# A retention layer with two mixers on one core: evictions of the up projection moved ahead of splits, two weight slots exchanged, one weight load moved ahead of the returning sum, first loads gated

## What is computed

```python
# retention, per head h
state = gamma[h] * state + outer(k[t], v[t]);  y[t] = scale * q[t] @ state
# mixer
theta = x @ w_theta
u = x + einsum('ts,bsd->btd', w_tok_r, x * cos(theta)) + einsum('ts,bsd->btd', w_tok_i, x * sin(theta))
x = u + maximum(u @ w_ch, 0)
# MLP
h = maximum(x.transpose(0, 2, 1) @ w_tok1, 0) @ w_tok2
u = x + h.transpose(0, 2, 1)
out = u + maximum(u @ w_ch1, 0) @ w_ch2          # d_ch = 1536
```

## Time and profile before

| | us |
|---|---|
| median of 3 runs | 440.97 (439.33 to 441.27) |
| the profiled execution | 443.38 |
| span of its trace, first to last instruction | 441.4 |
| TensorE busy in that span | 423.1 |
| VectorE busy | 309.3 |
| ScalarE busy | 179.0 |
| GpSimd busy | 115.6 |

### The profile page before, as it was taken

One profiled execution on the slowest core, in us unless ns is written; L12 is line 12 of the kernel. 1 busy time (PEld: TensorE's weight loads), 2 busy tenths in 40 slices (PEclk: granted clock), 3 DMA queues, 4 the chain that ended last, 5 costly groups with the idle time before them and its releaser, 6 DMA issues.

```text
span 441.4 us, 7037 instructions
## 1 busy us (share of the span) xinstructions
PE 423.1 (96%) x2820; PEld 399.6 (91%) x2820; DVE 309.3 (70%) x428; ACT 179.0 (41%) x273; POOL 115.6 (26%) x107
## 2 busy tenths in 40 slices
PE   6899999999999999999999979988999969999997
PEld 4687887899999999999989969989999959999997
DVE  2699997889999995244417872658456459999951
ACT  1336653654354546111312356133336163555500
POOL 1422240100210005996520035297341000000000
PEclk9999999999999999999999998999999999999999
DMA  8946779520495012001010600010023945530111
GB/s 300 405 153 252 299 174 234 108 72 25 120 209 196 6 46 96 2 31 65 0 49 15 246 26 0 1 48 1 0 73 113 314 108 97 126 103 9 63 71 73
DMA packets 12480, 47.78 MB, mean 108 GB/s; under 512 B 1185, under 2 KB 3361, under 8 KB 10657
## 3 DMA queue, kind: packets, MB, share of 16 engines
q1 hardware_dynamic: 9488, 33.03, 20.1%
q0 software_dynamic: 2816, 14.16, 14.4%
q10 hardware_dynamic: 144, 0.14, 0.1%
HBM read 41.04 MB, written 6.29 MB: 107 GB/s over the span
## 4 chain that ended last, share of the span: by engine, by line
PE 87%; DVE 5%; DMA 4%; ACT 2%; issue 2%; DVEq 0%; ACTq 0%
PE ps L1236 76%; PE ps L1253 3%; PE ps L1293 3%; DMA w_raw<-ch 3%; PE ps L1307 2%; PE ps L1384 1%; PE ps L1267 1%; DVE h_ops_c L1138 1%; DMA qkv_in<-qkv 1%; PE ps L1283 1%; DVE prob L882 1%; DVE u_sum L1065 1%; ACT u_a L751 0%; ACT u_b L751 0%; DVE w_sq L866 0%
## 5 line engine op out<-in xcount | busy, mean ns | idle before, releaser
L1236 PE MATMUL ps<-tw,zs 128*128 128x384 f32 x504 | 88.1, 335 | 0.0
L1236 PEld LDWEIGHTS ps<-tw,zs 128*128 128x128 f32 x504 | 87.4, 188 | 0.1
L1236 PE MATMUL ps<-h_ops_c,w_even 128*128 128x384 f32 x288 | 50.6, 334 | 0.0
L1236 PEld LDWEIGHTS ps<-h_ops_c,w_even 128*128 128x128 f32 x288 | 50.0, 188 | 0.0
L1236 PE MATMUL ps<-u_a,w 128*128 128x384 f32 x210 | 41.2, 340 | 4.0 <-DVE h_a L1107 3.1
L1236 PEld LDWEIGHTS ps<-u_a,w 128*128 128x128 f32 x210 | 37.2, 191 | 4.5 <-issue 4.5
L1236 PE MATMUL ps<-u_b,w 128*128 128x384 f32 x210 | 40.7, 339 | 0.0
L689 ACT ACTIVATE zs<-z 128x768 fp32r<-128x768 f32 x28 | 23.7, 846 | 36.9 <-PE ps L1236 36.9
L1236 PEld LDWEIGHTS ps<-u_b,w 128*128 128x128 f32 x210 | 37.6, 192 | 0.0
L1236 PE MATMUL ps<-ut,w_sq 128*128 128x384 f32 x192 | 35.5, 338 | 0.0
L1236 PEld LDWEIGHTS ps<-ut,w_sq 128*128 128x128 f32 x192 | 33.0, 188 | 0.0
(11 more groups left out here) (142 smaller groups left out, 781.7 us busy)
## 6 DMA issues: line engine op xcount, KB each, us to landing
qkv_in<-qkv SPq DMA_DIRECT2D x11, 1024.0 KB, 6.5
raw<-tok POOLq DMA_DIRECT2D x7, 1152.0 KB, 9.2
stage<-weights SPq DMA_DIRECT2D x11, 512.0 KB, 3.3
w_raw<-ch POOLq DMA_DIRECT2D x6, 768.0 KB, 6.8
cols_out<-res SPq DMA_DIRECT2D x2, 1536.0 KB, 5.2
total<-cols_out SPq DMA_DIRECT2D x4, 768.0 KB, 10.5
cols_out<-total SPq DMA_DIRECT2D x16, 192.0 KB, 1.8
raw<-tok SPq DMA_DIRECT2D x6, 384.0 KB, 7.1
```

The costliest lines, as they stand in the source:

```text
L1236: mm = pe.matmul(dst, left(l), right(r), start=first and n == 0, stop=last and n == 2, skip_group_check=True)
```

## The change

Line numbers behind the first hunk shift by a few; names are used from here on.

- **Evictions ahead of splits.** On VectorE, `sum_u(0, 3)` comes before `u_low(0, 4)`; in the first pair `sum_u(1, 2)` moves behind both `add_p7`; in every pair `second_units(m, 0, 1)` moves behind `add_p7` and `second_units(m, 1, 1)` behind `add_p2`. On ScalarE, `u_high(0, 5)` moves ahead of `keep_p1`, `u_high(1, 0)` ahead of `keep_p5`, and `u_high(1, 4)`, `(1, 5)`, `(1, 6)` behind both `first_units(m, 1, 1)`.
- **Operands of the down projection.** `h_op(0, 0)` is made at the start of pair 2 and `h_op(0, 1)` at the start of pair 3, each with its `h_sums(5, phi)`; before, both stood in the middle of pair 2 on ScalarE and at its start on VectorE. `h_sums(5, 2)` and `(5, 3)` move from the last pair into the first down product. `h_op_high(0, 0)` and `(0, 1)` get a wait on `u_lo[1]`, GpSimd's five splits.
- **Slots.** The slices of `w1` change places, and so do `w2_even` and `w2_odd`. With that `w2_raw1` lies over a part of the last slice's weights that only its products j = 1 and 2 read.
- **Second down weights.** SP loads `w2_raw1` after j = 2 of the last pair, ahead of the four blocks of `total`.
- **First loads.** SP waits for q and k of chunk 0 before it issues `theta_w`, for k and v of chunk 0 before chunk 2, and for chunk 1 before the third of `tok`.

```diff
--- before.py
+++ after.py
@@ -183,9 +183,9 @@
             u_b1 = sb("u_b1", [P, 4, 2, S], F32R, within=middle)
 
 
+        w2_odd = sb("w2_odd", [P, 2, W2C], F32R)
+        w2_raw1 = sb("w2_raw1", [P, W2C])
         w2_even = sb("w2_even", [P, 2, W2C], F32R)
-        w2_raw1 = sb("w2_raw1", [P, W2C])
-        w2_odd = sb("w2_odd", [P, 2, W2C], F32R)
         w2_raw0 = sb("w2_raw0", [P, W2C])
         total = sb("total", [P, B, NK, S])
 
@@ -238,7 +238,7 @@
             return hidden_units(row, phi, b)[:, half * HS:(half + 1) * HS]
 
         def w1_home(phi):
-            return w1_x[:, :, :] if phi == 2 else w1[:, (1, 0, None, 1, 0, 1)[phi], :, :]
+            return w1_x[:, :, :] if phi == 2 else w1[:, (0, 1, None, 0, 1, 0)[phi], :, :]
 
         def u_op(b, o):
             return u_a[:, o] if b == 0 else u_b1[:, o] if o < 4 else u_b2[:, o - 4]
@@ -479,11 +479,17 @@
             sp.dma_start(qkv_in[:, 0, 2 * DM:4 * DM], qkv[0, :, 2 * DM:4 * DM]).then_inc(chunk_in[0], 16)
             sp.dma_start(cst[:, C_OUT:N_CONST], consts[:, C_OUT:N_CONST]).then_inc(decay_in, 16)
             load_chunk(1)
+
+            sp.wait_ge(first_qk_in, 16)
             for i in range(2):
                 at = slice(i * THETA_HALF, (i + 1) * THETA_HALF)
                 sp.dma_start(raw[:, 0, at], theta_w[:, at]).then_inc(theta_in[i], 16)
             for g in range(2, NG):
+                if g == 2:
+                    sp.wait_ge(chunk_in[0], 16)
                 load_chunk(g)
+                if g == 2:
+                    sp.wait_ge(chunk_in[1], 16)
                 if g < 8:
                     load_third(g - 2)
 
@@ -499,14 +505,15 @@
 
             split_done(sp, N_PIECES - 1)
             sp.dma_start(w2_raw(0), ch2[1]).then_inc(w2_in[0], 16)
+
+            sp.wait_ge(up_ready, up_count(len(UNITS) - 1, 2))
+            sp.dma_start(w2_raw(1), ch2[0]).then_inc(w2_in[1], 16)
             for b in range(B):
                 sp.wait_ge(spilled[b], 16)
             sp.wait_ge(up_ready, up_count(len(UNITS) - 1, 3))
             for b, r in ((0, 0), (1, 1), (1, 0), (0, 1)):
                 sp.dma_start(total[:, b, 2 * r:2 * r + 2, :],
                              out[b, 2 * r:2 * r + 2].rearrange("k p s -> p k s")).then_inc(back[b][r], 16)
-            sp.wait_ge(up_ready, len(UNITS) * UP)
-            sp.dma_start(w2_raw(1), ch2[0]).then_inc(w2_in[1], 16)
             for p, r, b in ((1, 0, 0), (4, 1, 1), (5, 1, 0), (6, 0, 1)):
                 for i in range(CELLS):
                     m, half = i // 2, i % 2
@@ -785,7 +792,10 @@
                     act.wait_ge(h_sum, H_SUMS.index(p) * NPHI + phi + 1)
                 else:
                     units_kept(act, row, phi, b)
-                if p == 0 and phi >= 2:
+                if p == 0 and phi < 2:
+
+                    act.wait_ge(u_lo[1], len(U_PLAIN))
+                elif p == 0:
                     act.wait_ge(up_ready, up_count(len(UNITS) - 2, phi - 2))
                 elif p == 1:
                     act.wait_ge(up_ready, len(UNITS) * UP)
@@ -798,7 +808,9 @@
                 if p == 0:
 
                     act.wait_ge(up_ready, up_count(len(UNITS) - 3, UP - 1))
-                elif p >= 2:
+                elif p == 1:
+                    act.wait_ge(up_ready, len(UNITS) * UP)
+                else:
                     act.wait_ge(down_ready, (p - 1) * CELLS)
                 act.activation(w2(p)[:, 0, :], w2_raw(W2_RAW[p]), ACT.Copy, scale=W2_SIGN[p]).then_inc(w2_hi, 1)
 
@@ -814,40 +826,38 @@
                 first = [m for m in (n, n + 1) if UNITS[m][1] == 0]
                 if pair == 0:
                     u_high(0, 4)
+                    u_high(0, 5)
+                elif pair == 2:
+                    h_op_high(0, 0)
+                elif pair == 3:
+                    h_op_high(0, 1)
                 keep_p1(n)
                 if last:
                     h_op_high(0, 2)
                 keep_p1(n + 1)
                 if pair == 0:
-                    u_high(0, 5)
                     u_high(0, 6)
-                if last:
+                    u_high(1, 0)
+                elif last:
                     w2_high(0)
                 keep_p5(n)
                 keep_p5(n + 1)
-                if pair == 0:
-                    u_high(1, 0)
-                elif last:
+                if last:
                     h_op_high(0, 3)
                 keep_p6(n)
                 keep_p6(n + 1)
                 if pair == 0:
                     for o in range(1, 4):
                         u_high(1, o)
-                elif pair == 2:
-                    h_op_high(0, 0)
-                    h_op_high(0, 1)
                 elif last:
                     h_op_high(0, 4)
                 for m in first:
                     first_units(m, 0, 1)
-                if pair == 0:
-                    u_high(1, 4)
-                    u_high(1, 5)
                 for m in first:
                     first_units(m, 1, 1)
                 if pair == 0:
-                    u_high(1, 6)
+                    for o in range(4, UP):
+                        u_high(1, o)
                 for m in first:
                     first_units(m, 0, 0)
                 for m in first:
@@ -1089,10 +1099,9 @@
             u_low(0, 3)
             keep_u2(1, 3, 4)
             sum_u(0, 2)
-            u_low(0, 4)
-            u_low(0, 5)
             sum_u(0, 3)
-            u_low(0, 6)
+            for o in range(4, UP):
+                u_low(0, o)
 
             def add_p3(n):
                 dve.wait_ge(up_ready, up_count(n, 3))
@@ -1177,40 +1186,37 @@
                     sum_u(1, 1)
                 elif pair == 2:
                     h_op_low(0, 0)
+                    h_sums(5, 0)
+                elif pair == 3:
                     h_op_low(0, 1)
+                    h_sums(5, 1)
                 elif last:
                     h_op_low(0, 2)
                     w2_low(0)
                     h_op_low(0, 3)
-                    h_op_low(0, 4)
                 add_p3(n)
                 add_p3(n + 1)
                 if pair == 0:
                     u_low(1, 3)
-                    sum_u(1, 2)
+                elif last:
+                    h_op_low(0, 4)
+                add_p7(n)
+                add_p7(n + 1)
                 for m in second:
                     second_units(m, 0, 1)
-                add_p7(n)
-                add_p7(n + 1)
                 if pair == 0:
+                    sum_u(1, 2)
                     sum_u(1, 3)
-                for m in second:
-                    second_units(m, 1, 1)
-                if pair == 2:
-                    h_sums(5, 0)
-                    h_sums(5, 1)
-                elif last:
-                    h_sums(5, 2)
                 add_p2(n)
                 add_p2(n + 1)
                 for m in second:
+                    second_units(m, 1, 1)
+                for m in second:
                     second_units(m, 0, 0)
-                if last:
-                    h_sums(5, 3)
                 for m in second:
                     second_units(m, 1, 0)
             h_op_low(0, 5)
-            later = {0: [(5, 4), (5, 5)], 1: [(4, 0), (4, 1), (4, 2)], 2: [(4, 3), (4, 4), (4, 5)],
+            later = {0: [(5, 2), (5, 3), (5, 4), (5, 5)], 1: [(4, 0), (4, 1), (4, 2)], 2: [(4, 3), (4, 4), (4, 5)],
                      3: [(6, 0), (6, 1), (6, 2)], 4: [(6, 3), (6, 4), (6, 5)]}
             for p in range(DOWN):
                 if p + 1 < DOWN:
```

## The result

| | before | with the change |
|---|---|---|
| median, us | 441.12 (439.33 to 441.41, 4 runs) | 424.70 (424.39 to 426.48, 4 runs) |
| profiled execution, us | 443.38 | 424.39 |
| its span, us | 441.4 | 422.5 |
| up projection starts at, us | 248.94 | 244.78 |
| up projection, us | 95.95 | 87.36 |

The ratio is 0.9644 with an interval of 0.9607 to 0.9681: 3.6% faster. Two of all executions, one of the kernel before (515.9 us of span) and the profiled one of `e9` (698.8), ran at a mean granted clock of 0.755 and 0.558 and stay out of the ratios and of the comparisons of spans.

A forecast was written before the change was run, and what follows sets the result against it. TensorE, busy 423.1 of 441.4 us, was taken to bound the kernel with its holes; closing 8.6 us in the up and 6.1 in the down projection takes the median 440.97 to 426.3, plus 0.3 for margins: 426.6 us, range 424.8 to 431.0.

The forecast's parts named there:

- The sum of the two stages: Up and down projection: TensorE's stops and the low clock behind them go, saving 8.6 and 6.1 us, together 14.7.
- The walk by start-to-start times: First pair: instruction times followed on VectorE and ScalarE, putting add_p7 at 260.7 and 261.1, 0.8 us early.
- The rival that VectorE loses the port there: First pair: GpSimd's u_low starts ahead of u_low(1, 3), TensorE loses 1.2 us, 427.9 in all; chance 0.17.
- keep_p5: First pair, before product j = 3: TensorE's wait for this eviction goes, 1.01 us.
- add_p7: First pair, before product j = 6: the stop of 3.35 us goes, and 1.65 us of low clock behind it.
- pair 2: Up projection, stop before add_p7's product in pair 2: goes once the h_op low parts move, 2.5 us.
- Down projection: Second down weights land before the stage, w2_low(1) ends 3.7 us into it, total's block arrives in time: 6.1 us saved.
- operands that drip in *and* the low clock: Second down product: its first 18 matmuls take 5.84 instead of 3.12 us for both reasons.
- The gates: First loads: SP's waits move nothing, taken as 0, bounds -0.8 and +1.0 us; costing 1.0 had chance 0.03.
- I take the same 14.7 off the median.: Last step, whole kernel: the trace's saving of 14.7 us taken off the median 440.97, giving 426.3.
- The 0.3 for tight margins: Whole kernel: 0.3 us added because three margins are 0.4 to 0.8 us and one will likely miss.
- the test I had named: Check after the run: the up projection starts within 1 us of 248.94.

The follow-up runs named there:

- e9: Kernel before plus four unread fp32 products in each of its two stops of 3 us: 439.55 us against 441.11, ratio 0.9961.
- e5: Kernel before with only the exchanged slots and the second down weights loaded ahead of the returning sum: 433.92 us, ratio 0.9847.
- e6: Changed kernel with slots and second down weights as before and no gates, so only the moved evictions and operands: 430.94 us, ratio 0.9778.
- e7: Changed kernel with sum_u(1, 2) put back ahead of both add_p7 on VectorE in the first pair: 426.53 us.
- e10: Changed kernel with the order edits ahead of keep_p5 undone (sum_u(0, 3), u_high(0, 5), u_high(1, 0)): 426.58 us.
- e8: Changed kernel with h_op(0, 0) and h_op(0, 1) made in the middle of pair 2 again, their h_sums in pair 3: 426.33 us.
- e12: Kernel before with unread products in both stops of 3 us, plus three more in the stop of pair 2: 438.29 us against 440.63, ratio 0.9947.
- e1: Kernel before with only the three gates (SP's waits among the first loads) added: 440.56 us against 440.51, ratio 0.9995.
- e2: Changed kernel without the three gates (SP's waits among the first loads): 424.41 us.
- e3: Kernel before with one more idle 128x128 product filling the wait for q and k, no gate: 440.41 us, ratio 0.9987.
- e4: Changed kernel with its two first idle products shortened from 128x512 to 128x384, opening a wait before q and k: 427.16 us.

## Why the prediction was right, and where it was off

**The sum of the two stages: right.** 8.6 and 6.1 us were forecast, and in the two profiles 8.59 and 6.10 came; the up projection is 87.36 us long (87.4 forecast) and no stop took the place of those removed. `e5` and `e6` show each half by itself.

**First pair.** The walk by start-to-start times held to a tenth. Counted from the stage's start, 4.16 earlier than in the trace I read, `u_low(1, 3)` was to start at 259.1 - 4.16 = 254.94 and did so at 254.96, 0.96 us long as before: VectorE did get through between two of GpSimd's `u_low` (timeline, VectorE and GpSimd):

```profile
253.21 4.42 POOL L585 TENSOR_TENSOR u_b<-u_sum,u_b 128x768 fp32r<-128x768 f32 x2 [33.28 <-ACT u_b L758]
...
254.96 0.96 DVE L1084 SCALAR_TENSOR_TENSOR u_b<-res,u_b 128x768 fp32r<-128x768 f32 x1 [0.72 <-ACT u_b L758]
255.84 1.01 DVE L1116 TENSOR_TENSOR h_a<-h_a,ps 128x384 f32<-128x384 f32 x2
256.76 1.68 DVE L1075 TENSOR_TENSOR u_sum<-res 128x768 f32<-128x768 f32 x1
```

Both `add_p7` end at 256.85, 0.4 us before their product is due (244.78 + 12.48 = 257.26). The rival that VectorE loses the port there (1.2 us, 0.17) did not come. `e7` shows what it would have been like, with one instruction more in front.

**The price of single edits.** I gave `keep_p5` 1.01, `add_p7` 3.35 + 1.65 and pair 2 2.5 us. These are the losses in before's order of events, and they add up to the right 8.6, but they are not what each edit is worth by itself: taken back alone, they make the up projection 2.08 (`e10`), 1.85 (`e7`) and 1.52 us (`e8`) longer, 5.45 together. The `add_p7` stop of before had two causes in a row, the late orders ahead of `keep_p5` and `sum_u(1, 2)`; and the stops that come back are 1.61 us at most, with no fall of the clock behind any of them.

**Down projection.** `w2_raw1` landed 4.4 us after its issue at 324.01, 3.7 before the stage began; `w2_low(1)` ended 3.7 us into the stage, as forecast (332.14 + 3.7 = 335.84; timeline):

```profile
324.01 0.33 SPq L510 DMA_DIRECT2D w_raw<-ch  x1
...
334.08 1.76 DVE L1165 SCALAR_TENSOR_TENSOR w_odd<-w_raw,w_odd 128x1536 fp32r<-128x1536 f32 x1 [0.25 <-ACT w_odd L815]
...
337.50 0.55 DVE L1177 TENSOR_TENSOR total<-total,ps 128x384 f32<-128x384 f32 x1
```

`total`'s first block took 6.3 us (6.0 in the earlier trace rows); VectorE asked for it at 5.4 us into the stage and got it. One step was wrong, though it changed no number: I put the 2.72 us of the slow 18 matmuls down to operands that drip in *and* the low clock. By `e12` it is the operands alone: at a clock of 1.00 the same 18 took 5.81.

**The gates: nothing**, as forecast (`e1`, `e2`).

**The 1.9 us that were off.** The step that failed is the last: "I take the same 14.7 off the median." The profiled execution is not the median one. It had a late rise of the clock at the start, which the median lacks, and fewer dips than the median's executions. The rest of the measured 16.4 us, 1.7, can be read from `e1`, whose profile is a typical execution of the kernel before: it starts the up projection at 244.75 like the changed kernel (244.78), is 10.26 us longer in the up and about 6.0 in the down projection, and 10.26 + 6.0 is the 16.2 by which the spans differ (438.7 and 422.5). So the term mis-sized is the up projection, 8.6 for a typical 10.3, and the missing 1.7 is the low clock behind the stop in pair 2, which the prediction had put at nothing because the one trace it read showed none. Other executions have a dip elsewhere instead: the profile of `e3`, with a span of 438.5, has none in pair 2 but starts the up projection 1.8 us later. That the median forecast lies within 1.9 us is in part luck: the same sum gave 426.7 us for the span of the trace, and 422.5 came, 4.2 less, because the late rise that I had not booked is in the trace and not in the median. The 0.3 for tight margins was also not called on. And the test I had named, a start of the up projection within 1 us of 248.94, failed by 4.16 us for the same reason: I took the start for typical, though its rows give 2.08 and 1.97 us for 16 matmuls where later rows of the same trace give 1.16 and 1.09 for the same work.

What stays open: why the clock rises early in one execution of the kernel before and late in another. The idle products' end against the arrival of q and k has a part in it (`e4`), but not alone: `e3` ran into the low clock again after its first 16 matmuls. Open as well is why the clock falls behind the stop in pair 2 in some executions only.

## What to carry to other kernels

Where one engine is busy 96% of the span, compute its pace from an unhindered stretch, subtract, and book every missing microsecond to a row; the sum of the holes then forecasts the stages' gain in that trace to a tenth, while the value of one edit among several has to be had by taking it back alone. Before a difference in the trace is subtracted from a median, look whether the profiled execution is a typical one: rows with doubled durations at its start and the number of clock dips tell. On an engine that works strictly in order, move what evicts a bank for the critical engine ahead of work that has slack, above all of work that a neighbour can block for a whole instruction.

## What the hardware showed that I had not expected

- In the profiles of before and `e4` the granted clock is written 1.00 throughout the first 15 us, though rows take twice as long (16 matmuls of 64x128: 2.08 against 1.16 us); in `e3` and `e12` a fall at 8 us is written (0.55, 0.56). The durations are the surer sign there.
- Shortening the two idle products at the start, so that TensorE stood 0.83 us before its first data, cost 2.5 us at the end. The Trainium skill, "TensorE: Matmul & The Clock Gate", section on the clock gate, says that the ramp varies from run to run and is under 1% of a typical span; 2.5 of 424 us is 0.6%, so the size agrees, but all six executions of `e4` were slower than the middle of the changed kernel, by 1.39 us or more, so the work ahead of the data has a hand in it.
- In the two projections the clock was low behind the stops of 3.1 to 3.3 us in every profile that had one unfilled and behind one of 2.74 (`e3`), behind the stop of 2.3 to 2.4 us in two of four (0.57 in `e1`, 0.53 in `e5`, not in before and `e3`), and behind none of 1.61 us or less. At the start it also fell behind waits of 1.52 and 1.53 us (`e3`, `e12`), and behind the same wait of 1.52 in `e6` it did not, so the length of a stop alone does not tell.
- Eight products that nobody reads made the kernel before 0.4% faster (`e9`), eleven 0.5% (`e12`), without removing a wait.
